# Gates and row numbers of a mixture-of-experts layer: scattered as pairs during the expert stage, in place of a gate table, a transpose and 24 gathers

## What is computed

```python
for t in range(S):                      # attention, per batch b and head h
    state = f[:, :, t, :, None] * state + einsum('bhd,bhe->bhde', k[:, :, t], v[:, :, t])
    y[:, :, t] = einsum('bhd,bhde->bhe', q[:, :, t], state)
x = y.transpose(0, 2, 1, 3).reshape(B * S, H * D)          # 3072 x 384

logits = xn @ en.T / tau                # xn, en: rows scaled to length one
expert_idx = argmax(logits, axis=1)
gate_w = softmax(logits)[arange(N), expert_idx]
for e in range(8):
    mask = expert_idx == e
    out[mask] = gate_w[mask, None] * (maximum(x[mask] @ w1[e], 0.0) @ w2[e])

result = ((out @ w_a) * (out @ w_b)) @ w_out               # 384 -> 1536 -> 384
```

## Time and profile before

| | |
|---|---|
| median of 3 runs | 848.17 us (847.51 to 850.58) |
| the profiled execution, its own time | 850.97 us |
| its span, first to last instruction | 849.3 us |
| busy: PE, PEld, DVE, ACT, POOL | 96%, 86%, 43%, 38%, 17% of the span |
| mean granted clock of PE | 0.972 of full speed |

### The profile page before, as it was taken

The page is one execution under the profiler, slowest core; times in us unless marked ns, Lnnn a source line. Parts: engine busy times, 40 slices in busy tenths (PEclk is TensorE's granted clock), DMA queues, the critical chain, the costliest instruction groups (busy, mean ns, idle before and its releaser), DMA issues.

```text
span 849.3 us, 14234 instructions
## 1 busy us (share of the span) xinstructions
PE 812.3 (96%) x5309; PEld 731.8 (86%) x5310; DVE 366.2 (43%) x597; ACT 319.9 (38%) x604; POOL 145.1 (17%) x209
## 2 busy tenths in 40 slices
PE   6999995699999999999699999999999999999998
PEld 4999984599999999998388888888888888888887
DVE  6787887656543645355153232232223213222121
ACT  5677773245443545354142231231222213122121
POOL 4444442311022102005600100010001001000101
PEclk9999996599999999999799999999999999999999
DMA  9767651566654455120000000000000000000000
GB/s 223 185 191 203 193 168 36 147 223 200 209 165 169 130 204 164 58 74 2 0 1 1 10 28 1 1 38 1 0 10 29 1 1 38 0 1 1 38 0 38
DMA packets 32457, 67.52 MB, mean 79 GB/s; under 512 B 12008, under 2 KB 21277, under 8 KB 31261
## 3 DMA queue, kind: packets, MB, share of 16 engines
q1 hardware_dynamic: 28060, 55.92, 21.8%
q0 software_dynamic: 4352, 11.03, 3.8%
HBM read 57.46 MB, written 9.47 MB: 79 GB/s over the span
## 4 chain that ended last, share of the span: by engine, by line
PE 94%; DVE 3%; issue 2%; DMA 1%; ACT 0%; POOL 0%; DVEq 0%; POOLq 0%
PE scores L1007 18%; PE low_banks L1007 17%; PE sums L1014 9%; PE high_banks L1014 9%; PE sums L959 8%; PE low_banks L948 6%; PE scores L948 6%; PE high_banks L959 4%; PE scores L802 3%; PE sums L818 3%; PE high_banks L791 3%; PE low_banks L777 2%; PE sums L809 2%; PE low_banks L785 1%; PE high_banks L829 1%
## 5 line engine op out<-in xcount | busy, mean ns | idle before, releaser
L566 POOL DMA_INDIRECT out<-out_sb,out_row x24 | 23.4, 975 | 403.6 <-ACT out_sb L748 397.8
L1007 PE MATMUL scores<-x_hi,wab_lo 128*128 128x512 f32 x216 | 86.2, 399 | 2.2 <-issue 2.2
L1007 PE MATMUL scores<-yT_lo,wab_hi 128*128 128x512 f32 x216 | 86.4, 400 | 1.2 <-issue 0.8
L1398 DVE TENSOR_TENSOR h<-low_banks,a_sb 128x512 f32<-128x512 f32 x36 | 24.9, 692 | 144.9 <-ACT a_sb L731 144.4
L1007 PE MATMUL scores<-x_hi,wab_hi 128*128 128x512 f32 x216 | 85.2, 395 | 0.9 <-issue 0.8
L1007 PE MATMUL low_banks<-x_hi,wab_lo 128*128 128x512 f32 x216 | 84.7, 392 | 0.0
L1007 PE MATMUL low_banks<-yT_lo,wab_hi 128*128 128x512 f32 x216 | 84.6, 392 | 0.0
L1007 PE MATMUL low_banks<-x_hi,wab_hi 128*128 128x512 f32 x216 | 84.1, 389 | 0.0
L1398 DVE TENSOR_TENSOR h<-scores,a_sb 128x512 f32<-128x512 f32 x36 | 24.9, 692 | 131.6 <-ACT a_sb L731 115.6
L731 ACT ACTIVATE a_sb<-low_banks 128x512 f32<-128x512 f32 x36 | 21.5, 597 | 150.5 <-PE low_banks L1007 134.3
L731 ACT ACTIVATE a_sb<-scores 128x512 f32<-128x512 f32 x36 | 21.5, 596 | 135.5 <-PE scores L1007 131.2
(11 more groups left out here) (219 smaller groups left out, 1876.2 us busy)
## 6 DMA issues: line engine op xcount, KB each, us to landing
w_raw<-in_w SPq DMA_DIRECT2D x8, 1536.0 KB, 6.8
w_raw<-in_w SPq DMA_DIRECT2D x32, 384.0 KB
tok<-in_tok SPq DMA_DIRECT2D x48, 192.0 KB, 3.2
qk_all<-in_chan SPq DMA_DIRECT2D x48, 192.0 KB, 3.3
xd<-xst SPq DMA_DIRECT2D x24, 192.0 KB, 1.9
wab_raw<-in_wab SPq DMA_DIRECT2D x6, 768.0 KB, 6.3
wout_raw<-in_wout SPq DMA_DIRECT2D x1, 1536.0 KB, 6.4
wout_raw<-in_wout SPq DMA_DIRECT2D x1, 768.0 KB, 4.3
```

Source lines behind the costliest of these rows:

```text
L1007: last_op = pe.matmul(bank[2 * i + m][:, :], w[:, KM * m + k, cols], moving, start=(k == 0 and w is wab_hi and x is not None), stop=(k == ...
L1398: dve.tensor_tensor(h2[i][:, :], bank[2 * i + 1][:, :], a_sb[i][:, :], ALU.mult).then_inc(h_ready, 1)
```

## The change

The gate no longer goes over a transpose and a table by token. DVE writes `pairs`, for each token its row number (as an integer) and its gate, side by side, and `place_row`, the row of `pair_table` in which the pair of that token belongs: with place = 128 i + p, row 24 p + i. POOL scatters the pairs, 24 indirect DMAs of 128 pairs of 8 bytes, in two lots of 12: one behind `gather_x(2)`, one behind `gather_x(3)`. Once all have landed, SP loads `pair_table` back with one DMA, as `placed` (each of 128 partitions reads one piece of 192 bytes), between the sixth and the seventh turn of its weight loads. The output scatter takes its row numbers from `placed`, and `gate2` is the square of its other column. The transpose, the copy, the table store, the 24 gathers and three waits go.

```diff
@@ SP @@
+        sp_eng.wait_ge(pairs_scattered, 16 * TILES)
+        sp_eng.dma_start(placed[:, :, :].rearrange("p i two -> p (i two)"),
+                         pair_table.rearrange("(p i) two -> p (i two)", p=P)).then_inc(placed_loaded, 16)
...
-        sp_eng.wait_ge(gate_copied, 1)
-        sp_eng.dma_start(gate_table.rearrange("(b c p) o -> c b (p o)", b=B, c=C),
-                         gate_rows[:, :]).then_inc(gate_stored, 16)
@@ POOL @@
-        for j in range(2, FULL):
+
+        def scatter_pairs(low, high):
+            for i in range(low, high):
+                pool.indirect_dma_start(out=pair_table, out_offset=bass.IndirectOffsetOnAxis(ap=place_row[:, i:i + 1], axis=0),
+                                        in_=pairs[:, i, :], in_offset=None).then_inc(pairs_scattered, 16)
+
+        gather_x(2)
+        pool.wait_ge(gate_ready, 1)
+        scatter_pairs(0, TILES // 2)
+        gather_x(3)
+        scatter_pairs(TILES // 2, TILES)
+        for j in range(4, FULL):
             gather_x(j)
...
-        pool.wait_ge(row_ready, 1)
-        pool.wait_ge(gate_stored, 16)
-        for i in range(TILES):
-            pool.indirect_dma_start(out=gate_by_place[:, i:i + 1], out_offset=None, in_=gate_table,
-                                    in_offset=bass.IndirectOffsetOnAxis(ap=out_row[:, i:i + 1], axis=0)).then_inc(gate_gathered, 16)
+        pool.wait_ge(placed_loaded, 16)
@@ PE @@
-        pe.wait_ge(gate_ready, 1)
-        pe.transpose(bank[7][0:TILES, 0:P], gate[:, :], ident[:, :]).then_inc(gateT_done, 1)
...
-                if f == 0:
-                    pe.wait_ge(gate_copied, 1)
@@ DVE @@
-        dve.reciprocal(gate[:, :], r["sm2"][:, :]).then_inc(gate_ready, 1)
-        dve.tensor_scalar(out_row[:, :], r["token"][:, :], -1.0, None, ALU.add).then_inc(row_ready, 1)
+        dve.tensor_scalar(pairs[:, :, 0].bitcast(i32), row_no[:, :], float(MIDDLE - 1), None, ALU.add)
+        link(dve.tensor_scalar(r["start"][:, :], r["start"][:, :], 1.0 / P, -1.0 / P, ALU.mult, ALU.add))
+        dve.scalar_tensor_tensor(out=place_row[:, :], in0=r["low"][:, :], scalar=float(TILES), in1=r["start"][:, :],
+                                 op0=ALU.mult, op1=ALU.add)
+        dve.reciprocal(pairs[:, :, 1], r["sm2"][:, :]).then_inc(gate_ready, 1)
...
-        dve.wait_ge(gateT_done, 1)
-        dve.tensor_copy(gate_rows[:, :], bank[7][0:TILES, 0:P]).then_inc(gate_copied, 1)
...
-        dve.wait_ge(gate_gathered, TILES * 16)
-        dve.tensor_tensor(gate2[:, :], gate_by_place[:, :], gate_by_place[:, :], ALU.mult).then_inc(row_ready, 1)
-        dve.wait_ge(row_ready, 2)
+        dve.wait_ge(placed_loaded, 16)
+        dve.tensor_tensor(gate2[:, :], placed[:, :, 1], placed[:, :, 1], ALU.mult).then_inc(row_ready, 1)
+        dve.wait_ge(row_ready, 1)
```

More of the change, by code:

```diff
@@ L86, in attention_moe_ffn @@
     token = sb("token", [P, TILES], i32)
-    out_row = sb("out_row", [P, TILES], i32)
+    place_row = sb("place_row", [P, TILES], i32)
+    pairs = sb("pairs", [P, TILES, 2])
+    placed = sb("placed", [P, TILES, 2])
     source = sb("source", [P, (NT - 1) * TB], i32)
-    gate = sb("gate", [P, TILES])
     gate2 = sb("gate2", [P, TILES])
-    gate_by_place = sb("gate_by_place", [P, TILES])
     tile_expert = sb("tile_expert", [P, NT], i32)
@@ L108, in attention_moe_ffn @@
     table = sb("table", [TILES, P], i32)
-    gate_rows = sb("gate_rows", [TILES, P])
     arena = cursor[0]
@@ L222, in attention_moe_ffn @@
     token_table = nc.dram_tensor("token_table", [TOKENS + T, 1], i32, kind="Internal").ap()
-    gate_table = nc.dram_tensor("gate_table", [TOKENS, 1], fp32, kind="Internal").ap()
+    pair_table = nc.dram_tensor("pair_table", [TOKENS, 2], fp32, kind="Internal").ap()
     v_heads = tok_in[:, 0:DM].rearrange("r (a e d) -> r a e d", a=HP, e=2)
@@ L267, in attention_moe_ffn @@
     groups_ready, next_loaded, later_loaded, row_ready = map(sem, ("groups_ready", "next_loaded", "later_loaded", "row_ready"))
-    gate_ready, gateT_done, gate_copied, gate_stored, gate_gathered = map(
-        sem, ("gate_ready", "gateT_done", "gate_copied", "gate_stored", "gate_gathered"))
+    gate_ready, pairs_scattered, placed_loaded = map(sem, ("gate_ready", "pairs_scattered", "placed_loaded"))
     w1_loaded = sem("w1_loaded")
@@ L565, in _ @@
                 pool.wait_ge(o_ready[t], u + 1)
-                pool.indirect_dma_start(out=out, out_offset=bass.IndirectOffsetOnAxis(ap=out_row[:, u * B + t:u * B + t + 1], axis=0),
+                pool.indirect_dma_start(out=out, out_offset=bass.IndirectOffsetOnAxis(ap=placed[:, u * B + t, 0:1].bitcast(i32), axis=0),
                                         in_=out_sb[:, t, :], in_offset=None).then_inc(out_written[t], 16)
@@ L759, in _ @@
         step(0)
-        act.wait_ge(row_ready, 2)
+        act.wait_ge(row_ready, 1)
         for u in range(1, C):
```

## The result

The changed kernel took 852.09 us (median of 20 runs, 847.41 to 857.44), the kernel before 848.46 us beside it (20 runs, 845.94 to 851.54). The ratio is 1.0048 with a 95% interval of 1.003 to 1.0066: slower by 0.5%, where 1.6% faster was forecast. The profiled execution of the changed kernel took 856.21 us, its span is 854.9 us.

A forecast was written before the change was run, and what follows sets the result against it. PE, busy for 96% of the span, was taken to bound the kernel. From the 848.17 us median, 13.65 us for the gathers and 0.11 for the transpose gave 834.4 us; range 832.5 to 850 us.

The forecast's parts named there:

- Part 1: Feed-forward stage: removing the 24 gate gathers gives back PE's whole stall, -13.65 us (bounds 0 and 13.65).
- The rival that had the stall belong to the code: Feed-forward stage: the stall isn't the gathers' and PE crawls there anyway, 848.1 us; chance 0.18.
- Part 2: Transpose, copy, table store and waits go: -0.11 us for PE's transpose before the first feature, 0 for the rest.
- Part 3: DVE before the first `h_lo`: two more instructions, 0.2 to 0.6 us, covered by 2.55 us of idle time: 0.
- Part 4: Expert stage: 24 scatters between row gathers, about 15 us of POOL per lot of 12, hidden: 0.
- part of it moves along: Expert stage: rows of 16 crawl past the fourteenth transfer, 3.7 us, 838.1 us (837 to 843); chance 0.10.
- scatters starve PE throughout: Expert stage: POOL's many small elements beside busy DMA cost 21.9 us, 856.3 us; chance 0.12.
- Part 5: SP's loading back of the pairs: 12 us of cover for an issue of about 0.35 us: 0.

The follow-up runs named there:

- e7: Kernel before with one plain transfer in place of the 24 gate gathers, stalling chip 1: 836.84 us against 848.12, ratio 0.9863.
- e8: Kernel before with pauses between its gate gathers, in effect lots of 12, 4, 4, 4, stalling chip 1: 835.19 us against 848.12, ratio 0.9839.
- e15: Kernel before with each gate gather waiting for the one before to land, stalling chip 4: 836.64 us against 846.88, ratio 0.9879.
- e17: Kernel before with its 24 gate gathers in two lots of 12, stalling chip 12: 836.31 us against 848.22, ratio 0.9844.
- e6: Kernel before unaltered, run for its profile on stalling chip 1: 846.45 us.
- e18: Kernel before with 24 plain POOL transfers of 128 x 4 bytes for the gate gathers, stalling chip 12: 836.54 us against 848.22, ratio 0.9854.
- e2: Changed kernel with one plain transfer in place of its 24 scatters, quiet chip 3: 836.26 us, ratio 1.0000 to the kernel before.
- e10: Changed kernel with one plain transfer in place of its 24 scatters, repeated on quiet chip 7: 836.41 us, ratio 0.9997 to the kernel before.
- e16: Changed kernel unaltered, against the kernel before on stalling chip 12: 849.17 us against 848.22, ratio 1.0027.
- e5: Changed kernel unaltered, against the kernel before on stalling chip 1: 852.01 us against 848.12, ratio 1.005.
- e14: Changed kernel with its scatters in six lots of four, stalling chip 4: 836.76 us against 846.88 for the kernel before, ratio 0.9867.

## Why the prediction was wrong

**Part 1, the gathers go: right in mechanism, some 2 us too large.** The stall at 407.91 us came from the row of gathers (e7, e8, e15, e17), and it vanished in the changed kernel. Its size of 13.65 us was that of one profiled execution; that of e6 has 12.2. Medians give 848.12 - 836.84 = 11.3 us (e7), and 10.2 to 12.9 us with the other kernels that have no long row (e8, e15, e17, e18). The rival that had the stall belong to the code (0.18) falls. The exit from the expert loop is the same in e7, without a stall; so the Trainium skill's rule on taken branches ("Runtime: NRT & Kernel Launch", "Instruction fetch mechanics"), which stood beside that rival, isn't what this stall comes from. The spacing of the gathers, given as 1.25 us, is 1.31 on average ((419.76 - 389.53) / 23); nothing hangs on it.

**Part 2, transpose, copy, store: right.** 0.11 us can't be seen; e2 and e10, without them, are at 1.0000 and 0.9997.

**Part 3, DVE: right.** Two more instructions were forecast at 0.2 to 0.6 us, covered by 2.55 us of idle time. DVE in order of time:

```profile
163.20 0.18 DVE L1375 TENSOR_SCALAR pairs<-row_no 128x24 int32<-128x24 f16 x1
163.29 0.17 DVE L1376 TENSOR_SCALAR r_start<-r_start 128x24 f32<-128x24 f32 x1
163.50 0.19 DVE L1377 SCALAR_TENSOR_TENSOR place_row<-r_low,r_start 128x24 int32<-128x24 f32 x1
163.61 0.29 DVE L1379 RECIPROCAL pairs<-r_sm 128x24 f32<-128x24 f32 x1
165.81 0.61 DVE L1331 SCALAR_TENSOR_TENSOR h_lo<-low_banks,h_hi 128x432 fp32r<-128x432 f32 x1 [1.91 <-ACT h_hi L673]
```

The idle time before the first `h_lo` fell from 2.55 to 1.91 us: 0.64 us of the cover was used.

**Part 4, the scatters at 0: the step that failed.** Its time for the first lot was right: from 188.11 to 203.72 us (188.2 to 203.2 forecast), 0.97 us an instruction; and the DMA engines bore the small writes. The second lot came at 224.73 in place of 214.6, since the row gathers ahead of it waited for a group that the first row had already made late. But the sum priced the scatters by POOL's time and by bandwidth alone. The cost that part 1 had just put on an unbroken row of POOL's indirect transfers was not applied to the new rows, except in two rivals. The rival "part of it moves along" saw the rows of 16, and counted their harm from the fifteenth transfer at 3.7 us, because PE's stall before began there. The measured loss was 19.7 us in the first profile and 10.9 in that of e16. By medians it was 15.2 us on chip 1 (852.01 - 836.84, e5 and e7) and 12.6 on chip 12 (849.17 - 836.54, e16 and e18). Two things were wrong in that count. PE's gaps were taken for the beginning, while ACT was late sooner. In the profile of before its product was due at 400.44, 11 us into the row, and came at 403.89:

```profile
403.89 0.60 ACT L731 ACTIVATE a_sb<-scores 128x512 f32<-128x512 f32 x1 [4.35 <-remote]
...
423.82 0.60 ACT L731 ACTIVATE a_sb<-low_banks 128x512 f32<-128x512 f32 x1 [16.27 <-remote]
```

And late work is passed on: in the expert stage ACT's lateness stops PE's up-projection, which reuses four banks, so PE waits for `h_lo` and for ACT, not for its own instructions alone. In the feed-forward stage there is more room: the 4.9 us in e17 cost nothing. The rival "scatters starve PE throughout" had the right place, the right sign and nearly the size of the first profile (21.9 us against 19.7), with a chance of 0.12. That was luck, as e16 and e5 lose 10.9 and 16.4 us, and its cause was wrong: it laid it on the many small elements, and lots of four with the same elements are harmless (e14). What it was refuted with, that row gathers in fours leave PE busy, said nothing about rows of 16.

**Part 5, loading back: right.** SP in order of time:

```profile
332.28 0.33 SPq L432 DMA_DIRECT2D placed<-pair_table  x1
344.09 0.34 SPq L418 DMA_DIRECT2D w_raw<-in_w  x1
```

11.8 us of cover, as forecast (12).

What stays open: what slows ACT and PE in a long row. That PE gets no instructions was inferred, from gaps inside runs of matmuls that wait for nothing. The one block of instructions that the prediction saw was fetched at about 393 us, ahead of the stall, and the next on that queue (q8) at about 432, after it; in e7, without a stall, blocks come at about 393 and 418. So a block that was fetched late isn't seen, and the trace doesn't name q8 as PE's. No run shows what POOL and the other engines share there, whether indirect transfers are needed, or why some chips, or times, show nothing. Every execution here had its spans and clocks recorded; whether the stall is there without that isn't known.

## What to carry to other kernels

When a stall has been put down to a kind of work, and the change moves work of that kind elsewhere, charge the new place with it first: here -13.65 us at one place became +19.7 us at another in the profiles, and about -11 became +15 by the medians of chip 1. Count a row of such transfers from its true start, with whatever stands ahead of it in the queue (4 + 12 = 16), and break it up: two rows of 12, or lots behind work that is there anyway, were free where one row of 24 cost 11 us. And look for the first engine that is late, not for the one whose gaps are largest: ACT was late in rows of 8 and 12 as well, and only the room behind it kept that from costing time.

## What the runs showed of the hardware

- Rows of back-to-back indirect transfers from POOL slow ACT and PE on some chips: 24 in 31 us cost 11.3 us by medians, two rows of 16 (21 us each) between 10.9 and 19.7 us in three profiles. Rows of 12 (16 us) and of 8 cost no time here, though ACT was 4.9 us late in one of 12 (e17) and 3.1 us in one of 8 (e14). The DMA engines were at 0.01 of their time in the stall of the kernel before, and at 0.02 as the first one of the changed kernel began.
- Whether this happens goes with the chip or the time of the run: the same kernel took 836.73 and 836.41 us on two chips, and 848.12, 846.88 and 848.22 us on three others.
- 24 plain transfers of 128 x 4 bytes took POOL 12.8 us, 24 indirect ones 31. The plain ones made neither ACT nor PE late on a stalling chip (e18); the indirect ones did, in a longer row.
